# Attention probabilities kept whole: one fp32 product on two column groups instead of two split products

## The reference

```
B, H, S, D = 2, 8, 768, 64          # 16 heads in all
q_assign, k_assign = argmax over 16 centroids of the normalised q and k
scores = scale * q @ k.T, and -1e9 where q_assign differs from k_assign
attn = exp(scores - max) / (sum + 1e-9)
out  = attn @ v                     # then the mixing and the two blocks
```

## Time and profile before

| | |
|---|---|
| median of 3 runs | 707.22 us (707.11 to 707.36) |
| the profiled execution's own time | 707.65 us |
| its span, first to last instruction | 705.8 us |
| PE busy | 694.2 us, 98% of the span |
| DVE, ACT, POOL busy | 53%, 44%, 36% |
| mean granted TensorE clock | 0.99 |

### The profile page before, as it was taken

One profiled execution on the slowest core, in us unless ns is written; L12 is line 12 of the kernel. 1 busy time (PEld: TensorE's weight loads), 2 busy tenths in 40 slices (PEclk: granted clock), 3 DMA queues, 4 the chain that ended last, 5 costly groups with the idle time before them and its releaser, 6 DMA issues.

```text
span 705.8 us, 10209 instructions
## 1 busy us (share of the span) xinstructions
PE 694.2 (98%) x3810; PEld 607.6 (86%) x3810; DVE 375.7 (53%) x710; ACT 309.5 (44%) x634; POOL 254.7 (36%) x280
## 2 busy tenths in 40 slices
PE   8899999999999999999999999999999999999998
PEld 7699889899999999888888888888888899988876
DVE  4898988979888856953113211131111489933410
ACT  4777777777778851311111111121111377743411
POOL 6756896696499132388600000000050070000000
PEclk7899999999999999999999999999999999999999
DMA  5453424434245021143200000010050520000011
GB/s 170 132 134 103 122 78 130 136 81 114 63 130 162 19 66 33 31 120 107 72 1 0 1 1 0 1 60 1 1 178 1 159 80 1 1 31 30 31 46 45
DMA packets 25921, 47.11 MB, mean 67 GB/s; under 512 B 3728, under 2 KB 10768, under 8 KB 25616
## 3 DMA queue, kind: packets, MB, share of 16 engines
q1 hardware_dynamic: 23392, 38.11, 19.2%
q0 software_dynamic: 2336, 7.95, 3.5%
q10 hardware_dynamic: 144, 0.39, 0.2%
HBM read 36.02 MB, written 3.15 MB: 55 GB/s over the span
## 4 chain that ended last, share of the span: by engine, by line
PE 92%; DVE 6%; ACT 1%; issue 1%; POOL 0%; DVEq 0%; ACTq 0%; POOLq 0%
PE ps L1590 19%; PE ps L1556 19%; PE ps L1352 10%; PE ps L1338 10%; PE ps L1638 9%; PE ps L1652 9%; PE ps L1327 5%; PE ps L1328 5%; PE ps L1362 3%; PE ps L1433 2%; PE ps L1282 1%; PE ps L1403 1%; PE ps L1488 1%; DVE pt_l L919 1%; PE ps L1575 1%
## 5 line engine op out<-in xcount | busy, mean ns | idle before, releaser
L1160 DVE SCALAR_TENSOR_TENSOR hid_l<-ps,hid_h 128x512 fp32r<-128x512 f32 x48 | 33.2, 692 | 197.1 <-ACT hid_h L806 197.1
L806 ACT ACTIVATE hid_h<-ps 128x512 fp32r<-128x512 f32 x48 | 28.8, 599 | 223.6 <-PE ps L1556 223.6
L919 DVE TENSOR_TENSOR pt_l<-ps,pt_h 128x384 fp32r<-128x384 f32 x192 | 106.0, 552 | 36.3 <-ACT pt_h L708 35.9
L708 ACT ACTIVATE pt_h<-ps 128x384 fp32r<-128x384 f32 x192 | 94.6, 494 | 37.0 <-PE ps L1338 36.8
L1338 PE MATMUL ps<-cst,prob 128*128 128x128 f32 x576 | 97.3, 278 | 2.3 <-DVE pt_l L919 1.2
L912 DVE TENSOR_REDUCE row_min<-ps 128x1 f32<-128x768 f32 x96 | 91.2, 950 | 2.3 <-PE ps L1328 2.3
L1338 PEld LDWEIGHTS ps<-cst,prob 128*128 128x128 f32 x576 | 69.3, 142 | 21.9 <-issue 14.3
L697 ACT ACTIVATE prob<-ps,row_min 128x768 f32<-128x768 f32 x96 | 86.5, 901 | 2.4 <-DVE row_min L912 2.4
L1590 PE MATMUL ps<-w_h,hid_h 128*128 128x512 f32 x192 | 76.2, 397 | 0.0
L1590 PE MATMUL ps<-w_h,hid_l 128*128 128x512 f32 x192 | 75.5, 393 | 0.0
L1590 PE MATMUL ps<-w_l,hid_h 128*128 128x512 f32 x192 | 74.7, 389 | 0.0
(11 more groups left out here) (179 smaller groups left out, 1515.0 us busy)
## 6 DMA issues: line engine op xcount, KB each, us to landing
w_raw<-in_moe_w_ch SPq DMA_DIRECT2D x24, 256.0 KB, 2.5
raw_d<-in_q SPq DMA_DIRECT2D x8, 384.0 KB, 3.3
raw_v<-in_v SPq DMA_DIRECT2D x16, 192.0 KB, 2.5
out<-out_s SPq DMA_DIRECT2D x12, 256.0 KB, 2.0
raw_qk<-in_k SPq DMA_DIRECT2D x15, 192.0 KB, 3.3
raw_qk<-in_q SPq DMA_DIRECT2D x15, 192.0 KB, 3.2
q<-q SPq DMA_DIRECT2D x15, 192.0 KB, 3.9
k<-k SPq DMA_DIRECT2D x15, 192.0 KB, 3.4
```

Source lines behind the costliest of these rows:

```text
L708: nc.scalar.activation(pt_h[a][:, R * hf:R * hf + R, (t % R) * P:(t % R + 1) * P], ps[:, 4 + hf, 0:HALF].rearrange("p (j c) -> p j c", j=R ...
L919: nc.vector.tensor_tensor(pt_l[a][part], ps[:, 4 + hf, 0:HALF].rearrange("p (j c) -> p j c", j=R), as_f32(pt_h[a][part]), ALU.subtract).th ...
```

## The change

The turned probabilities are no longer split. ACT stores the left half of a turned tile (keys 0 to 383) and DVE the right half, each once, in plain fp32, into `pt`, of which there are now two sets (head parity). v is loaded straight into one of three buffers `v_n` in fp32; `split_v` on POOL is gone. `values` has one fp32 product for each key block, with 64 stationary columns; even blocks use the lower 64 columns of the array and rows 0 to 63 of the bank, odd blocks the upper ones. The two parts of a half have four and two key blocks instead of three and three. `step` now makes the scores first and then both turns. In head 0, fourteen products of zeros are put between the steps.

```
-                for j in range(R * part, R * part + R):
-                    for src in (pt_h[a], pt_l[a]):
-                        last = nc.tensor.matmul(ps[:, o_bank(n, a), 0:HALF], v_n[s][:, j, :, :], src[:, j, :],
-                                                start=j == 0 and src is pt_h[a],
-                                                stop=j == NT - 1 and src is pt_l[a])
+                for j in ((0, 1, 2, 3), (4, 5))[part]:
+                    at = D * (j % 2)
+                    last = nc.tensor.matmul(ps[at:at + D, o_bank(n, a), 0:HALF], v_n[n % V_BUFS][:, j, :],
+                                            pt[n % 2][a][:, j, :], start=j < 2, stop=j >= NT - 2)
...
             def turn(n, t, hf):
...
                 if g:
-                    pe.wait_ge(low_ready, 2 * g - 1 + hf)
+                    pe.wait_ge((left_stored, right_stored)[hf], g)
...
             def step(n, s, t):       # PE
-                turn(n, t, 0)
                 if t < 4:
                     scores(n, s, t + 2)
                 else:
                     scores(n + 1, 1 - s, t - 4)
+                turn(n, t, 0)
                 turn(n, t, 1)
...
             def step(n, s, t, more=True):       # ACT
-                store_high(n, t, 0)
                 if t < 5:
                     exponent(n, s, t + 1)
                 elif more:
                     exponent(n + 1, 1 - s, 0)
-                store_high(n, t, 1)
+                store_left(n, t)
...
             def step(n, s, t, more=True):       # DVE
-                store_low(n, t, 0)
                 if t < 4:
                     minimum(n, s, t + 2)
                 elif more:
                     minimum(n + 1, 1 - s, t - 4)
-                store_low(n, t, 1)
+                store_right(n, t)
...
             def store_right(n, t):
                 g, a = 6 * n + t, t // R
+                dve.wait_ge(turn_ready, 2 * g + 2)
+                if t % R == 0 and n >= 2:
+                    dve.wait_ge(o_ready, AHEAD + 2 * (n - 2) + a + 1)
+                nc.vector.tensor_copy(pt[n % 2][a][:, R:2 * R, (t % R) * P:(t % R + 1) * P],
+                                      ps[:, 5, 0:HALF].rearrange("p (j c) -> p j c", j=R)).then_inc(right_stored, 1)
...
             def load_v(i, s):
+                n = 2 * i + s
+                if n >= V_BUFS:
+                    sp.wait_ge(o_ready, AHEAD + 2 * (n - V_BUFS) + 2)
...
             scores(0, 0, 1)
+            keep_busy(2, 6)
             dots(1)
+            keep_busy(2, 6)
             step(0, 0, 0)
             turn_dots(1)
+            keep_busy(2, 6)
             step(0, 0, 1)
+            keep_busy(3, 6)
             step(0, 0, 2)
+            keep_busy(2, 6)
             turn_mask(1)
+            keep_busy(1, 6)
             step(0, 0, 3)
```

More of the change, by code:

```diff
@@ L115, in build @@
         prob = [sb(att, f"prob{s}", [NT, P]) for s in range(2)]
-        pt_h = [sb(att, f"pt_h{a}", [NT, HALF], F32R) for a in range(2)]
-        pt_l = [sb(att, f"pt_l{a}", [NT, HALF], F32R) for a in range(2)]
+        pt = [[sb(att, f"pt{par}{a}", [NT, HALF]) for a in range(2)] for par in range(2)]
+        v_n = [sb(att, f"v_n{j}", [NT, D]) for j in range(V_BUFS)]
         o_s = sb(att, "o_s", [HALF])
@@ L184, in build @@
         cst_loaded, cen_loaded = sem("cst_loaded"), sem("cen_loaded")
-        q_loaded, k_loaded, v_loaded = sem("q_loaded"), sem("k_loaded"), sem("v_loaded")
+        q_loaded, k_loaded = sem("q_loaded"), sem("k_loaded")
+        v_loaded = [sem(f"v_loaded{j}") for j in range(V_BUFS)]
         q2_copied = [sem(f"q2_copied{s}") for s in range(2)]
@@ L913, in minimum @@
                                         axis=AX.XY, op=ALU.min).then_inc(min_ready, 1)
-            def store_low(n, t, hf):
+            def store_right(n, t):
                 g, a = 6 * n + t, t // R
[L917 to L920, removed]
+                dve.wait_ge(turn_ready, 2 * g + 2)
+                if t % R == 0 and n >= 2:
+                    dve.wait_ge(o_ready, AHEAD + 2 * (n - 2) + a + 1)
+                nc.vector.tensor_copy(pt[n % 2][a][:, R:2 * R, (t % R) * P:(t % R + 1) * P],
+                                      ps[:, 5, 0:HALF].rearrange("p (j c) -> p j c", j=R)).then_inc(right_stored, 1)
             def first_masks(j):
@@ L1345, in values @@
                 if part == 0:
-                    pe.wait_ge(low_ready, 12 * n + 6 * a + 6)
-                    pe.wait_ge(v_split, n + 1)
+                    for stored in (left_stored, right_stored):
+                        pe.wait_ge(stored, 6 * n + 3 * a + 3)
+                    pe.wait_ge(v_loaded[n % V_BUFS], 16 * (n // V_BUFS + 1))
                     if 2 * n + a:
                         pe.wait_ge(x_stored, AHEAD + 2 * n + a - (o_bank(n, a) == 7))
[L1350 to L1354, removed]
+                for j in ((0, 1, 2, 3), (4, 5))[part]:
+                    at = D * (j % 2)
+                    last = nc.tensor.matmul(ps[at:at + D, o_bank(n, a), 0:HALF], v_n[n % V_BUFS][:, j, :],
+                                            pt[n % 2][a][:, j, :], start=j < 2, stop=j >= NT - 2)
                 if part == 1:
@@ L1398, in _, with keep_busy @@
             pe.sem_inc(fold_ready, AHEAD)
[L1399 removed]
+            def keep_busy(count, bank=5):
                 blank = cen_b[:, :, :].rearrange("p a b -> p (a b)")
                 for _ in range(count):
[L1403 removed]
+                    nc.tensor.matmul(ps[:, bank, 0:P], blank, blank, start=True, stop=True)
             pe.wait_ge(cen_cleared, 1)
```

73 lines of the change are left out of this document (30 added, 43 removed).

## The result

The changed kernel takes **713.02 us** (median of 5 runs, 711.08 to 714.13) against 707.36 us of the kernel before beside it (707.11 to 709.67). The ratio is 1.0071, 95% interval 1.005 to 1.0092: it is slower by 3.5 to 6.5 us. Forecast were 705.9 us and a slight gain; the time lies 0.02 us beyond the upper edge of the range, 713. The profiled execution was the fastest of the five, 711.08 us with a span of 709.2, 3.4 us over that of before.

What follows compares the result with a forecast made beforehand. PE was taken to bound the kernel. Products of `values` +10.8, waits -9.6 and head 0 -2.5 summed to -1.3 us, so the profiled 707.65 became 706.35 and the median forecast 705.9 us; range 697 to 713.

Steps and rivals of the forecast that it cites:

- What bounds the kernel: Whole kernel: PE carries 92% of the chain that ended last and bounds the attention; waiting is 0.64 us a head.
- The products of `values`: PE in `values`: 192 narrow fp32 products replace 384 at 68.0 us and take 78.8 us, 10.8 us more.
- S: PE in `values`: distance of two sets of narrow-product records, between 0.320 and 0.347 us, taken as 0.33.
- E: PE around each narrow detour: cost of entering and leaving the narrow form, taken as 0.27 us, for 57 detours.
- The waits: PE waits in the 15 heads behind head 0: all 0.64 us a head goes, -9.6 us.
- Head 0: Start of the kernel: lighter DVE and fillers keep the clock at 1.00; taken as -2.5 us.
- the bound of +0.5: Head 0: the slower end of its forecast change in us; the other end was -3.2.
- The waits did not stay: Slower rival: PE's turns wait for ACT's left store behind the exponential; 715.5 us if nothing gained; chance 0.14 for at least half staying.
- Weights do load under a running product: Slower rival in `values`: each of 192 products shows its 0.108 us load, +20.7 us, 726.6 us; chance 0.07.
- 0.43 was the sign: Sign in `values`: the prediction is wrong if sets stand 0.43 us apart; 0.32 to 0.35 was expected.
- Passes do not hold up the other group: Slower rival in `values`: two passes delay the other column group, each part one set later, +19 us, 724.7 us; chance 0.07.
- The cheaper way in and out: Faster rival in `values`: entering and leaving costs only 0.13 us, 8 us less, 697.9 us; chance 0.20.

Runs made afterwards that it cites:

- the joined version: Changed kernel with the two parts of each half joined into one stretch of narrow products, 32 stretches in all; 708.96 us, ratio 1.002 to the kernel before.
- the best version: Changed kernel with both parts of each half joined at the place of the first part, without fillers; 705.43 us, ratio 0.9971 to the kernel before.

## Why the prediction was wrong

*What bounds the kernel* was right: PE, before and after.

*The products of `values`* was the step that failed, in the size of a term. The forecast was +10.8 us. Measured, a head has 2 x (1.64 + 1.00) = 5.28 us against 4.25. In six heads a part stands in front of `dots`: from 124.34, when the transposes of 123.69 are done, to 126.11 (0.177 ahead of the product at 126.29) the two take 1.77 us, so the part adds 0.84 to the 0.93 of `dots`. In six others one leads to the mask's transposes, for 0.05 less, and in the last head two parts join. Over 16 heads that is 82.8 us against 68.0, about +14.9.

S was taken as 0.33 and is 0.322, which is 1.5 us less. **E was taken as 0.27 and is 0.355: 57 x 0.085 = 4.8 us more.** It was read from `dots`, whose first set is 0.024 us longer than its second, where here it is 0.051 (a term that the working named and left out of the sum), and the exit was read before transposes, where `values` mostly leads to scores: 0.10 us late there (122.88 to 123.16), 0.06 before transposes. And a part in front of `dots` was taken to pay nothing for the change: 0.64 us, its two sets. It pays 0.20 more, over six heads 1.2 us. 10.8 - 1.5 + 4.8 - 0.3 (seven ways out before transposes) + 1.2 = 15.0.

The Trainium skill (TensorEngine Tiling (Array Packing), Key Properties) says that a change of the tiling mode, and not just of the tile, drains the engine. The runs agree in so far as each change costs time, 0.35 to 0.38 us for the way in and out; no row shows the draining itself.

*The waits* was right. None is left in the steady heads: two heads are 0.63 us longer with 1.85 us more in `values` (one head with `dots`, one with the mask), so 0.61 us a head went, where 0.64 were read. Over 15 heads that is 9.2 us for a forecast of 9.6. The cause that was given fits the run with the old order of PE and ACT, which has no waits either; the second set of `pt` and DVE's new order were not told apart from it.

*Head 0* gained 1.7 us up to the second `dots` in the first profile, and 0.2 in the second (34.10, 32.44 and 33.91 us). In it are 0.5 us more for the two parts of `values` that stand there, so its own gain is 2.2 or 0.7 us, where 2.5 were forecast. The reason given was wrong for the greater part: the clock stays up without fillers, and in the kernel before the fillers gain nothing, though the clock stays up with them. Their price was too high as well, 14 x 0.22 = 3.1 us for twelve that make 2.6, and the bound of +0.5 has no working.

The sum with measured terms: 14.9 - 9.2 - 0.7 to 2.2 = +3.5 to +5.0 us. The ratio says +3.5 to +6.5.

*The rivals.* The waits did not stay, though they came back where two steps follow each other without anything between, in the joined version by 0.48 us a head of the 0.61 that had been saved. Weights do load under a running product of the same rows: four loads start between 121.4 and 121.5 us, where only two records start, which run to 121.98, and of the 20.7 us that uncovered loads would have cost nothing shows (S of 0.322 where 0.43 was the sign). Passes do not hold up the other group. The cheaper way in and out, which had been given 0.20, was the opposite of what happened. Why a change of form costs just this stays open: the rows show where the 0.355 us lie, and not how much of it is an unhidden load.

## What to carry to other kernels

Two half-width products side by side save nothing if each pair is fenced in by full-width work. Here a pair in a long stretch costs 0.644 us and the four full-width products that it replaces 0.71, a gain of 0.064 a pair; a way in and out at 0.355 eats that of between five and six pairs (an estimate from these rows), and a stretch had one to three. So count the changes of form, price one by a product put inside a stretch and one put ahead of it, and gather narrow products into few long stretches. Then look at what stood between the pieces, since the engines that feed PE used that time; where the stretch is placed was worth 3 to 4 us here. And when the work of a second reader of a bank went, PE's waits went with it, in both orders tried; that, and not the narrow products, is what the best version gains by.

## What the runs showed that was not expected

- Two column groups took their products independently of their order in the program: 0, 2, 1, 3 costs the same 1.5 us as 0, 1, 2, 3.
- Going from narrow products of 64 columns to narrow ones of 32 (`dots`) takes 0.79 us from the start of a one-pair part, as going back to full width does (132.90 to 133.70). What is spared is the 0.10 us ahead of the next narrow stretch and the 0.10 behind the first: part and `dots` together take 1.77 us.
- Executions of the same program differ by 3 us (711.1 to 714.1). Of the two that have a profile, 2.5 us apart, 1.5 lie in the first 33 us, with steady heads equal to 0.01 us; half clock lasted 6.9 us in one and 10.3 in the other.
- The fillers of head 0 multiply `cen_b`, which by then holds the centroids, so they are not products of zeros.
- In the profile of the kernel before with the fillers the column of the granted clock reads 1.00 throughout the start, though a score product of 384 columns at 16.78 us lasts 0.52 us, as at half clock, and 0.34 from 22 us on. The length of the products tells what the column missed.
